# Stacked 128-row attention scores from copies in SBUF, and an earlier, partly moved conversion of q and k

## Chip, cores and metric

One core of one Trainium2 chip. The time is device microseconds of one execution; the kernel before takes 1062.03 us, the median of 3 runs (1060.99 to 1062.84).

## The reference

Three stages follow one another. Attention with 4 sink keys and a window of 128, over 4 batches x 8 heads x 768 positions x 64; an MLP with g = h - tanh(h); a mixture of 8 experts, of which each token takes one.

```python
scores = scale * np.matmul(q, k.transpose(0, 1, 3, 2))
keep = is_sink | in_window                 # 4 sink keys, and 0 <= i - j < 128
a = softmax(np.where(keep, scores, -1e9))
x = a @ v                                  # tokens 3072 x 512
h = x @ w_in;  y = (h - np.tanh(h)) @ w_out          # 512 -> 2048 -> 512
e = argmax(y @ w_gate + bias); out = gate * (relu(y @ w1[e]) @ w2[e])
```

## The kernel before

Every float32 product is made of float16 parts: x = hi + lo, and a product is lo*hi + hi*lo + hi*hi, accumulated in PSUM. Before the split, q and k of a group are scaled by a power of two found from their largest magnitude per partition (`qk_top_of`, L394: a reduction on VectorE; `qk_scales`, L405: eight small integer operations on VectorE, each followed by a wait for it; `qk_multiply`, L424: GpSimd multiplies in place; `conv`, L433: ScalarE writes hi, GpSimd writes lo = raw - hi).

Work is counted in pairs r = 0 to 95: one block of 128 queries of two heads. The two heads lie on partitions 0 to 63 and 64 to 127. Three pairs make a group g = r // 3 (384 queries), four groups a chunk of 384 tokens, and eight chunks are the whole; chunk m is also the token block of MLP window m. Each pair runs through `score_pair` (L566: six matmuls of 64 rows, three for each head, into two PSUM banks; VectorE masks and takes the maximum; ScalarE takes the exponential), `normalise`, `gather_sinks` (every third pair), `transpose_probs`, `transpose_sinks` (every third pair), `weigh_values` (64-column value products) and `split_x`. A block is 132 or 260 key columns wide: 132 where a sequence begins.

Pairs 0 to 13 are made in `alone` (L1270), two counts i = 2r and 2r + 1 for each pair, with the preparation of values and MLP weights (`prepare_alone`, L1171) between them. From pair 14 on they stand beside the MLP: `window` (L1315) has 32 slots k; even slots hold the first product of a hidden block (`mlp_in`, L756) and a pair, odd slots the second product (`mlp_out`, L816); four even slots of each window hold no pair. `between` puts the scores of a pair into the middle of the first product, after its xt_lo part. In window m the router of chunk m - 1 is worked (`gate_slot`, L963), the first part of its rank chain in slot 22.

`conversions` (L1154) says at which count i = 2r + (k mod 2) a group's reductions, scale and splits are issued. Groups 1 to 4 have counts of their own, group g from 5 on 6g - 9 (q top), 6g - 7 (k top, scale, multiply), 6g - 5 (q split), 6g - 3 (k split); its first pair is at count 6g. All engines run in order; every hand-over is a semaphore. SyncE (SP) issues the loads in the order written in `loads` (L1376): load_qk(g) waits until group g - 2 is converted, then in some places a value load with six small sink loads, or the store of a finished chunk.

Of the kernel before, what the change touches and what calls it, by code (L numbers as in the profile page):

```python
# [59 lines left out]
STRIP = 32  # L60
RING = 2
# [43 lines left out]
def attention_buffers(sb):  # L105
# [3 lines left out]
    k_hi, k_lo = ([sb(f"k_{x}{s}", [P, KR], F16) for s in range(2)] for x in ("hi", "lo"))  # L109
    v_raw = sb("v_raw", [P, NB2, DM], F32)  # L110
# [8 lines left out]
    words = 2 * QK + 2 * CT + 2 * KR + NB2 * DM + 2 * NB2 * HP * VW + 2 * DM + 2 * RING * KB + 6 * KB + 4 * SINK + P + 27 * P + 2 * RING * P  # L119
    return (qk_raw, q_hi, q_lo, k_hi, k_lo, v_raw, v_hi, v_lo, vs_raw, vs_all, probs, normed, sinks, pt, merged), words  # L120


def front(nc, dram, shared, attention):

    with ExitStack() as ctx:
# [6 lines left out]
        (qk_raw, q_hi, q_lo, k_hi, k_lo, v_raw, v_hi, v_lo, vs_raw, vs_all, probs, normed, sinks, pt,  # L132
# [35 lines left out]
        qk_top = sb("qk_top", [P, 2], F32)  # L168
# [22 lines left out]
        def h_of(m, f):  # L191
# [3 lines left out]
                 "qk_scaled qk_mult conv_hi conv_lo sink_zero sink_copied "  # L195
# [198 lines left out]
        def qk_top_of(E, eng, a, hp, i):  # L394

            g = HP * a + hp
            if E == "dve":
                if i == 0:
                    eng.wait_ge(q[f"qk_in{g % 2}"], 16 * (g // 2 + 1))
                elif g == 0:  # L400
                    eng.wait_ge(q["first_k_in"], 16)
                exponent_step(eng, eng.tensor_reduce(qk_top[:, i:i + 1], qk_raw[g % 2][:, qk_cuts(a)[i]], AX.X, ALU.max,  # L402
                                                     apply_absolute_value=True))

        def qk_scales(E, eng, a, hp):  # L405

            g = HP * a + hp
            if E == "dve":
                need(eng, q["qk_mult"], 2 * (g - 2))
                s = qk_scale[:, g % 2, :]  # L410
                for i in range(2):
                    one_exp = qk_exp[:, i:i + 1]
                    exponent_step(eng, eng.tensor_scalar(one_exp, qk_top[:, i:i + 1].bitcast(I32), 255 * EXP1, None,
                                                         ALU.bitwise_and))
                    exponent_step(eng, eng.tensor_scalar(one_exp, one_exp, float(LOWEST * EXP1), float(HIGHEST * EXP1),
                                                         ALU.max, ALU.min))
                exponent_step(eng, eng.tensor_scalar(qk_half[:], qk_exp[:, 1:2], qk_exp[:, 0:1], 0.5,
                                                     ALU.subtract, ALU.mult))
# [1804 lines left out]
```

## Time and profile before

| | |
|---|---|
| median of 3 runs | 1062.03 us |
| profiled execution, whole | 1065.34 us |
| its span, first to last instruction | 1063.4 us |
| TensorE (PE) busy | 979.7 us, 92% |
| VectorE (DVE) busy | 649.2 us, 61% |
| ScalarE (ACT) busy | 533.0 us, 50% |
| GpSimd (POOL) busy | 413.3 us, 39% |
| mean granted TensorE clock | 0.970 |

The profiled execution is 3.3 us above the median of the runs. PE's matmuls are pipelined: a row's duration overlaps the next row's, so the distance between starts tells what a matmul costs, not its duration. "PEld" are its weight loads.

### The profile page before, as it was taken

What the parts mean: (1) busy time and instruction counts of PE and PEld (TensorE: products, weight loads), DVE (VectorE), ACT (ScalarE), POOL (GpSimd) and SP (SyncE); (2) the same over time, 40 slices, a digit from 0 to 9 for tenths busy, and PEclk for the clock granted to TensorE, in tenths of its full rate; (3) what the DMA queues carried; (4) which work ended last, traced back from release to release, by engine and by line L of the source; (5) the groups of instructions that cost most, each with busy time, mean ns of one, the idle gap of its engine ahead of it and who ended that gap; (6) DMA issues with size and microseconds to landing.
All of it is one profiled execution on the core that took longest, in us unless ns stands there. A gap on an engine that the chain in (4) does not pass through costs nothing.

```text
span 1063.4 us, 23350 instructions
## 1 busy us (share of the span) xinstructions
PE 979.7 (92%) x7808; PEld 591.2 (56%) x7808; DVE 649.2 (61%) x1824; ACT 533.0 (50%) x1329; POOL 413.3 (39%) x605
## 2 busy tenths in 40 slices
PE   3647999999999999999999999999899999899996
PEld 2423444554554555555455455555576777677773
DVE  7565877767768767777866765547574324733331
ACT  4454776655646764655665555446512224522221
POOL 4555887524325533434642432200132322232322
PEclk9666999999999999999999999999999999999998
DMA  9502001102100212101110100051115112111111
GB/s 349 183 18 79 19 18 36 49 19 81 64 19 19 48 37 79 49 19 36 19 48 19 36 31 1 2 188 31 24 29 208 50 50 45 40 41 49 50 50 38
DMA packets 24371, 60.26 MB, mean 57 GB/s; under 512 B 9504, under 2 KB 9760, under 8 KB 22752
## 3 DMA queue, kind: packets, MB, share of 16 engines
q1 hardware_dynamic: 15392, 45.77, 13.2%
q0 software_dynamic: 5728, 13.43, 4.1%
q8 instruction: 44, 0.72, 0.3%
q10 hardware_dynamic: 3168, 0.02, 0.2%
q14 instruction: 39, 0.32, 0.1%
HBM read 45.35 MB, written 14.12 MB: 56 GB/s over the span
## 4 chain that ended last, share of the span: by engine, by line
PE 70%; DVE 14%; issue 5%; ACT 4%; POOL 3%; DMA 2%; DVEq 1%; ACTq 0%; POOLq 0%; SPq 0%
PE h_ps L772 18%; PE acc L828 18%; PE pt_ps L1897 5%; PE h_ps L1948 5%; PE acc L1948 5%; PE s_ps L1897 5%; PE s_ps L579 3%; PE x_out L727 3%; PE pt_ps L646 2%; PE s_ps L879 2%; DVE g_raw L793 1%; ACT probs L602 1%; ACT g_hi L803 1%; PE s_ps L772 1%; DVE qk_top L402 1%
## 5 line engine op out<-in xcount | busy, mean ns | idle before, releaser
L828 PE MATMUL acc<-w_out_all,g_hi 128*128 128x512 f16 x768 | 228.4, 379 | 0.0
L772 PE MATMUL h_ps<-xt_hi,w_in_all 128*128 128x384 f16 x960 | 197.5, 329 | 5.4 <-DVE g_raw L793 3.5
L828 PE MATMUL acc<-w_out_all,g_lo 128*128 128x512 f16 x384 | 146.0, 380 | 2.7 <-DVE g_lo L813 2.7
L772 PEld LDWEIGHTS h_ps<-xt_hi,w_in_all 128*128 128x128 f16 x960 | 91.0, 100 | 65.2 <-issue 8.6
L784 ACT ACTIVATE g_raw<-h_ps,batch_scale 128x384 f32<-128x384 f32 x120 | 69.6, 580 | 101.8 <-PE h_ps L772 101.8
L102 POOL TENSOR_TENSOR tick<-tick 1x1 f32<-1x1 f32 x83 | 15.5, 187 | 264.8 <-ACT y L1964 117.1
L828 PEld LDWEIGHTS acc<-w_out_all,g_hi 128*128 128x128 f16 x768 | 75.2, 98 | 77.7
L813 DVE SCALAR_TENSOR_TENSOR g_lo<-g_raw,batch_scale,g_hi 128x384 f16<-128x384 f32 x128 | 88.4, 690 | 41.9 <-ACT g_hi L803 40.5
L803 ACT ACTIVATE g_hi<-g_raw,batch_scale 128x384 f16<-128x384 f32 x128 | 79.0, 617 | 60.7 <-DVE g_raw L793 59.0
L661 POOL TENSOR_SCALAR_AFFINE_SELECT pt<-merged 128x512 f16<-128x512 f16 x96 | 65.3, 680 | 91.6 <-DVE merged L655 89.8
L772 PE MATMUL h_ps<-xt_lo,w_in_all 128*128 128x384 f16 x480 | 99.0, 329 | 0.0
L793 DVE SCALAR_TENSOR_TENSOR g_raw<-h_ps,batch_scale,g_raw 128x384 f32<-128x384 f32 x120 | 74.0, 617 | 38.4 <-ACT g_raw L784 35.7
L619 ACT ACTIVATE normed<-probs,row_sum 128x132 f32<-128x132 f32 x192 | 66.8, 395 | 31.0 <-DVE row_sum L613 22.2
L651 ACT ACTIVATE merged<-pt_ps 128x256 f16<-128x256 f32 x96 | 36.6, 382 | 75.7 <-PE pt_ps L646 75.2
L602 ACT ACTIVATE probs<-s_ps,neg_max 128x132 f32<-128x132 f32 x192 | 68.6, 365 | 6.4 <-DVE neg_max L596 6.2
L430 POOL TENSOR_SCALAR qk_raw<-qk_raw,qk_scale 128x384 f32<-128x384 f32 (+2 forms) x62 | 37.6, 618 | 75.1 <-DVE qk_scale L421 75.1
L772 PEld LDWEIGHTS h_ps<-xt_lo,w_in_all 128*128 128x128 f16 x480 | 47.4, 99 | 31.9 <-issue 1.4
L1861 ACT ACTIVATE xg<-xg,x_scale 128x512 f32<-128x512 f32 x23 | 16.6, 722 | 94.2 <-DVE x_undo L1858 94.2
L594 DVE COPY_PREDICATED s_ps<-later,s_ps 128x256 f32<-128x256 int32 x80 | 34.2, 428 | 47.6 <-PE s_ps L579 46.2
L451 POOL TENSOR_TENSOR q_lo<-qk_raw,q_hi 128x384 f16<-128x384 f32 x31 | 29.0, 934 | 83.5 <-ACT q_hi L447 83.4
L828 PEld LDWEIGHTS acc<-w_out_all,g_lo 128*128 128x128 f16 x384 | 37.5, 98 | 40.2 <-issue 5.2
L579 PE MATMUL s_ps<-k_hi,q_lo 64*128 64x260 f16 (+1 forms) x192 | 27.5, 282 | 31.0 <-ACT probs L602 21.7
(314 smaller groups left out, 2203.3 us busy)
## 6 DMA issues: line engine op xcount, KB each, us to landing
qk_raw<-in_qk SPq DMA_DIRECT2D x31, 454.0 KB, 3.3
raw<-in_w SPq DMA_DIRECT2D x16, 512.0 KB, 7.8
v_raw<-in_v SPq DMA_DIRECT2D x4, 1536.0 KB, 7.0
x_tokens<-x SPq DMA_DIRECT2D x24, 256.0 KB, 2.5
w_in_all<-in_w_in SPq DMA_DIRECT2D x4, 1024.0 KB, 8.8
w_out_all<-in_w_out SPq DMA_DIRECT2D x4, 1024.0 KB, 11.0
x_tokens<-g_raw SPq DMA_DIRECT2D x1, 1024.0 KB, 6.4
vs_raw<-in_v SPq DMA_DIRECT2D x24, 4.0 KB
```

The source lines that it names most:

```text
L579: mm = eng.matmul(s_banks[j][:, cols], l[s][rows, t * P:(t + 1) * P], k[s][rows, t * KB + cols.start:t * KB + KW], start=(i == 0), stop=(i ...
L602: eng.activation(probs[:, r % RING, j, :], s_banks[j][:, P:KW], ACT.Exp, bias=neg_max[:, r % RING, j:j + 1], scale=1.0, accum_out=row_sum[ ...
L619: eng.activation(normed[:, 2 * t + j, :], probs[:, r % RING, j, :], ACT.Copy, scale=row_sum[:, r % RING, j, 0:1])\
L661: eng.affine_select(out=at[:, :, 1, :], in_=both, pattern=[[0, 4], [1, P]], compare_op=ALU.is_ge, fill=0.0, base=0, channel_multiplier=-1) ...
L772: mm = eng.matmul(h_of(m, f), w16[0][:, f, x * DM + k * P:x * DM + (k + 1) * P], r[:, par, k, :], start=(i == 0), stop=(i == 3 * KD - 1))
L784: eng.activation(g_raw[:, f % 2, :], h_of(m, f), ACT.Tanh, scale=batch_scale[:, b, 0:1]).then_inc(q["tanh_done"], 1)
L793: eng.scalar_tensor_tensor(g, h_of(m, f), batch_scale[:, b, 0:1], g, ALU.mult, ALU.subtract).then_inc(q["g_done"], 1)
L803: eng.activation(g_hi[f % 2][:], g, ACT.Copy, scale=batch_scale[:, b, 1:2]).then_inc(q["g_hi_done"], 1)
L813: eng.scalar_tensor_tensor(g_lo[f % 2][:], g, batch_scale[:, b, 1:2], g_hi[f % 2][:], ALU.mult, ALU.subtract)\
L828: mm = eng.matmul(acc[t][:, :], l[f % 2][:, t * P:(t + 1) * P], w16[1][:, f, x * DM:(x + 1) * DM], start=(f == 0 and i == 0), stop=(f == N ...
L1897: mm = eng.matmul(hid_ps[c][:, (f - 4 * c) * P:(f - 4 * c + 1) * P], w[:, k, f * P:(f + 1) * P], x[p][:, k * P:(k + 1) * P], start=(i == 0 ...
L1948: mm = eng.matmul(y_ps[bank][:, :], l[:, f * P:(f + 1) * P], rhs, start=(f == 0 and i == 0), stop=(f == KF - 1 and i == 2))
```

## The change

Scores: from group 5 on (`STACKED = 5`) the operands are stacked to 128 rows, q as (q_hi, q_lo), the keys as (k_hi, k_hi) and (k_lo, k_lo). Two full-array matmuls for each head then give all four products, instead of three of 64 rows. The stacks are made by 12 DMA copies inside SBUF for each group, issued by SP before load_qk(g + 2). Conversions: the counts are earlier. Scale: qk_scales has five instead of eight operations, and runs on GpSimd for all groups but the first; qk_top has two buffers. In the alone part the value work moves: value scale and multiply earlier, value split and sink work later, weight Gram from count 5, sink transposes of ScalarE and VectorE one count later, first value products of a group one pair later in two places.

```diff
+STACKED = 5
+        q_stack = [sb(f"q_stack{s}", [P, 2, CT], F16) ...]; kh_stack, kl_stack: [P, 2, KR]
 def qk_top_of
-                exponent_step(eng, eng.tensor_reduce(qk_top[:, i:i + 1], ...))
+                need(eng, q["qk_scaled"], g - 1)
+                eng.tensor_reduce(qk_top[:, g % 2, i:i + 1], ...).then_inc(q["qk_topped"], 1)
 def qk_scales
-            if E == "dve":            # 8 operations, [P, 1] each
+            if E == ("pool" if g else "dve"):
+                step = chain(eng, q["qk_step"], QK_STEPS * g)
+                eng.wait_ge(q["qk_topped"], 2 * (g + 1))
+                need(eng, q["qk_mult"], 2 * (g - 2))
+                step(eng.tensor_scalar(qk_exp[:], qk_top[:, g % 2, :].bitcast(I32), 1.0 / EXP1, float(LOWEST), ALU.mult, ALU.max))
+                step(eng.tensor_scalar(qk_exp[:], qk_exp[:], float(HIGHEST), 0.0, ALU.min, ALU.add))
+                step(eng.tensor_scalar(qk_half[:], qk_exp[:, 1:2], qk_exp[:, 0:1], 0.5, ALU.subtract, ALU.mult))
+                step(eng.tensor_scalar(s[:, 0:1].bitcast(I32), qk_half[:], 127.0, float(EXP1), ALU.add, ALU.mult))
                 eng.tensor_scalar(s[:, 1:2]...).then_inc(q["qk_scaled"], 1)
+def stack_qk(E, eng, g):                # on SP
+                eng.wait_ge(q["conv_lo"], 2 * (g + 1))
+                eng.wait_ge(q["scores"], TPC * (g - 1))
+                for hh in range(2):
+                    for dst, part in (... six: q_hi, q_lo, k_hi twice, k_lo twice; 64 rows each ...):
+                        eng.dma_start(dst, part).then_inc(q[f"stacked{s}"], 16)
 def sink_halves
-                    eng.wait_ge(q["qk_mult"], 6)
+                    eng.wait_ge(q["conv_lo"], 8)
 def score_pair
+                if t == 0 and g >= STACKED:
+                    eng.wait_ge(q[f"stacked{s}"], stacked(g))
+                    for j in range(2):
+                        for i, k in enumerate((kl_stack, kh_stack)):
+                            mm = eng.matmul(s_banks[j][:, cols], q_stack[s][:, 1 - j, t * P:(t + 1) * P],
+                                            k[s][:, 1 - j, t * KB + cols.start:t * KB + KW], start=(i == 0), stop=(i == 1))
 def conversions
-                early = {1: (None, 0, 1, 2), 2: (4, 5, 7, 8), 3: (8, 9, 11, 12), 4: (14, 15, 17, 18)}
-                ... early.get(g, (6 * g - 9, 6 * g - 7, 6 * g - 5, 6 * g - 3))
+                early = {1: (None, 0, 1, 2), 2: (4, 5, 6, 7), 3: (8, 9, 10, 11), 4: (13, 14, 15, 16), 5: (19, 20, 21, 22)}
+                ... early.get(g, (6 * g - 11, 6 * g - 9, 6 * g - 7, 6 * g - 6))
 def prepare_alone
-            spread (PE) i == 5; v_scales, v_multiply 6; v_split 7; sink_multiply 8; sink_halves 9; weight_gram 4, 6, 7, 8
+            spread (PE) i == 4; v_scales 4 (DVE), v_multiply 5; v_split 8; sink_multiply 9; sink_halves 11; weight_gram 5, 6, 7, 8
 def alone
-            weighed = {5: (1,), 6: (2,), 7: (4, 5)}      # r: pairs weighed; (r - 2,) from 8 on
+            weighed = {5: (1,), 7: (2,), 8: (4, 5)}      # (r - 2,) from 9 on
+                    if i == 2 * r + (E in ("act", "dve")):   # was i == 2 * r for all
+                        stage(transpose_sinks, E, eng, r - 1)
 def loads
+                if g - 2 >= STACKED:
+                    stack_qk("sp", eng, g - 2)
                 load_qk("sp", eng, g)
+            stack_qk("sp", eng, HP * NC - 2)
+            stack_qk("sp", eng, HP * NC - 1)
```

## Rows read from the trace of the kernel before

**Rows 1.** Windows view: stretch, length, busy PE, PEld, DVE, ACT, POOL, clock, DMA.

```profile
8.40:88.40 80.00, 40.75 (x332) 27.30 (x332) 52.73 (x173) 41.45 (x131) 44.98 (x63) 0.72 0.47 176
88.40:187.00 98.60, 90.19 (x580) 44.77 (x580) 73.44 (x180) 65.90 (x171) 71.79 (x84) 0.95 0.08 25
187.00:765.00 578.00, 565.22 (x3767) 309.50 (x3764) 398.71 (x1114) 333.75 (x877) 209.94 (x290) 1.00 0.13 41
```

**Rows 2.** Timeline of PE, second window: start us, length, line, out<-in, shapes, count.

```profile
240.71 0.81 PE L772 MATMUL h_ps<-xt_lo,w_in_all 128*128 128x384 f16 x4
241.46 0.28 PE L579 MATMUL s_ps<-k_hi,q_lo 64*128 64x260 f16 x2
...
241.89 0.44 PE L646 MATMUL pt_ps<-ident,normed 128*128 128x128 f32 x2
...
245.61 0.81 PE L772 MATMUL h_ps<-xt_lo,w_in_all 128*128 128x384 f16 x4
246.26 0.38 PE L646 MATMUL pt_ps<-ident,normed 128*128 128x128 f32 x2
246.48 0.81 PE L772 MATMUL h_ps<-xt_hi,w_in_all 128*128 128x384 f16 x4
247.23 0.30 PE L727 MATMUL x_out<-pt,v_hi 128*64 128x256 f16 x2
...
250.26 0.52 PE L680 MATMUL pt_ps<-ident,sinks 128*128 128x128 f32 x3 [1.12 <-DVE merged L655]
...
250.83 0.59 PE L828 MATMUL acc<-w_out_all,g_hi 128*128 128x512 f16 x2
251.57 0.66 PE L772 MATMUL h_ps<-xt_hi,w_in_all 128*128 128x384 f16 x3
```

**Rows 3.** Timeline of PE: first score row of pairs 25, 27 and 30.

```profile
177.47 0.28 PE L579 MATMUL s_ps<-k_hi,q_lo 64*128 64x260 f16 x2
...
186.87 0.23 PE L579 MATMUL s_ps<-k_hi,q_lo 64*128 64x132 f16 x2
...
209.56 0.23 PE L579 MATMUL s_ps<-k_hi,q_lo 64*128 64x132 f16 x2
...
209.83 0.82 PE L772 MATMUL h_ps<-xt_hi,w_in_all 128*128 128x384 f16 x4
```

**Rows 4.** Timeline of PE's weight loads, alone stage at full clock.

```profile
54.65 0.92 PEld L293 LDWEIGHTS acc<-w_out_all 128*128 128x128 bf16 x16
```

**Rows 5.** SP's issue of six small loads; DMA view: size, us to landing.

```profile
243.83 2.36 SPq L472 DMA_DIRECT2D vs_raw<-in_v  x6
...
qk_raw<-in_qk SPq DMA_DIRECT2D x1, 192.0 KB, 2.4
slots<-table_fill SPq DMA_DIRECT2D x1, 192.0 KB, 6.9
```

**Rows 6.** Timeline of DVE: first and last of a group's eight scale operations.

```profile
246.84 0.15 DVE L413 TENSOR_SCALAR qk_exp<-qk_top 128x1 int32<-128x1 int32 x1
...
248.22 0.15 DVE L421 TENSOR_SCALAR qk_scale<-qk_scale 128x1 int32<-128x1 int32 x1
```

**Rows 7.** Waits of PE, 200 to 700 us, then 88 to 200: total, times, longest.

```profile
PE pt_ps L680 <- DVE merged L655: 5.0, 5, 1.1
...
PE pt_ps L680 <- DVE merged L655: 3.8, 4, 1.5
```

**Rows 8.** Groups of POOL by form: busy us, mean ns.

```profile
L102 POOL TENSOR_TENSOR tick<-tick 1x1 f32<-1x1 f32 x83 | 15.5, 187 | 264.8 <-ACT y L1964 117.1 <-DVE payload L951 66.7 <-DMA slot_g<-slots 40.4
...
L263 POOL TENSOR_SCALAR mod<-mod 128x24 f32<-128x24 f32 x1 | 0.4, 389 | 0.1
```

**Rows 9.** Timeline of ACT and POOL in the alone stage.

```profile
28.58 1.96 ACT L508 ACTIVATE v_hi<-v_raw 128x512 f16<-128x512 f32 x3 [1.94 <-POOL v_raw L493]
...
30.71 3.39 POOL L511 TENSOR_TENSOR v_lo<-v_raw,v_hi 128x512 f16<-128x512 f32 x3
...
36.29 0.63 ACT L525 ACTIVATE vs_all<-vs_raw 128x512 f16<-128x512 f32 x1 [3.04 <-POOL vs_raw L517]
```

More of the change, by code:

```diff
@@ L109, in attention_buffers @@
     k_hi, k_lo = ([sb(f"k_{x}{s}", [P, KR], F16) for s in range(2)] for x in ("hi", "lo"))
+    q_stack = [sb(f"q_stack{s}", [P, 2, CT], F16) for s in range(2)]
+    kh_stack, kl_stack = ([sb(f"k{x}_stack{s}", [P, 2, KR], F16) for s in range(2)] for x in ("h", "l"))
     v_raw = sb("v_raw", [P, NB2, DM], F32)
@@ L118, in attention_buffers @@
     merged = sb("merged", [P, RING, 2, 2, P], F16)
-    words = 2 * QK + 2 * CT + 2 * KR + NB2 * DM + 2 * NB2 * HP * VW + 2 * DM + 2 * RING * KB + 6 * KB + 4 * SINK + P + 27 * P + 2 * RING * P
-    return (qk_raw, q_hi, q_lo, k_hi, k_lo, v_raw, v_hi, v_lo, vs_raw, vs_all, probs, normed, sinks, pt, merged), words
+    words = 2 * QK + 4 * CT + 6 * KR + NB2 * DM + 2 * NB2 * HP * VW + 2 * DM + 2 * RING * KB + 6 * KB + 4 * SINK + P + 27 * P + 2 * RING * P
+    return (qk_raw, q_hi, q_lo, k_hi, k_lo, q_stack, kh_stack, kl_stack, v_raw, v_hi, v_lo, vs_raw, vs_all, probs, normed, sinks, pt, merged), words
 def front(nc, dram, shared, attention):
@@ L131, in front @@
         xt_hi, xt_lo = (sb(n, [P, 2, KD, CT], F16) for n in ("xt_hi", "xt_lo"))
-        (qk_raw, q_hi, q_lo, k_hi, k_lo, v_raw, v_hi, v_lo, vs_raw, vs_all, probs, normed, sinks, pt,
+        (qk_raw, q_hi, q_lo, k_hi, k_lo, q_stack, kh_stack, kl_stack, v_raw, v_hi, v_lo, vs_raw, vs_all, probs, normed, sinks, pt,
          merged) = attention
@@ L455, in conv, with stacked @@
                        .then_inc(q["conv_lo"], 1)
+        def stack_qk(E, eng, g):
+            s = g % 2
+            a = g // HP
+            k = key_cols(a)
+            if E == "sp":
+                eng.wait_ge(q["conv_lo"], 2 * (g + 1))
+                eng.wait_ge(q["scores"], TPC * (g - 1))
+                for hh in range(2):
+                    of_head = slice(D * hh, D * hh + D)
+                    upper, lower = slice(0, D), slice(D, P)
+                    for dst, part in ((q_stack[s][upper, hh, :], q_hi[s][of_head, :]),
+                                      (q_stack[s][lower, hh, :], q_lo[s][of_head, :]),
+                                      (kh_stack[s][upper, hh, k], k_hi[s][of_head, k]),
+                                      (kh_stack[s][lower, hh, k], k_hi[s][of_head, k]),
+                                      (kl_stack[s][upper, hh, k], k_lo[s][of_head, k]),
+                                      (kl_stack[s][lower, hh, k], k_lo[s][of_head, k])):
+                        eng.dma_start(dst, part).then_inc(q[f"stacked{s}"], 16)
+        def stacked(g):
+            return 16 * 12 * ((g - STACKED) // 2 + 1)
         def load_v(E, eng, b):
@@ L1280, in alone @@
                         score_pair(E, eng, r + 1)
[L1281 removed]
+                    for of in weighed.get(r, (r - 2,) if r > 8 else ()):
                         stage(weigh_values, E, eng, of)
@@ L1297, in alone @@
                         conversions(E, eng, i)
+                    if i == 2 * r + (E in ("act", "dve")):
+                        stage(transpose_sinks, E, eng, r - 1)
                     if i == 2 * r:
-                        stage(transpose_sinks, E, eng, r - 1)
-                        for of in weighed.get(r, (r - 2,) if r > 7 else ()):
+                        for of in weighed.get(r, (r - 2,) if r > 8 else ()):
                             stage(split_x, E, eng, of)
```

48 lines of the change are left out of this document (20 added, 28 removed).

## Prediction, made before the changed kernel was run

> **What bounds the kernel now.** I read the page first for the shares of the engines, then the windows view, which makes stages of the span [rows 1]: 8.4 to 88.4 us, 14 pairs scored "alone" (TensorE, PE, busy 40.8 of 80 us at a granted clock of 0.72); 88.4 to 187 us, the first MLP window (90.2 of 98.6); 187 to 765 us, the other windows (565.2 of 578 at full clock); then the experts, which the change leaves. In the windows a nanosecond off PE's own queue is a nanosecond off the span, and one off VectorE (DVE) counts only where PE waits for it. In the alone stage PE's own length hardly matters; the round trip ACT, PE, DVE does.
>
> Next PE's timeline in a window. A pair's scores stand between two parts of a hidden block. With them the transposes start 1.18 us after the xt_lo row (240.71 to 241.89); a slot later, without them, 0.65 us after (245.61 to 246.26) [rows 2]. So one pair's scores cost 0.53 us. The four matmuls of 384 columns in those 0.65 us give 0.423 ns a column, so 260 columns are 0.11 us; six such in 0.53 us cannot run one after another (0.66): the two 64-row halves run side by side, three passes, 0.33 us. The other 0.20 us is two pauses of 0.10: 240.71 + 0.65 = 241.36 against a first score at 241.46, and 241.46 + 0.33 = 241.79 against transposes at 241.89. The same pause stands ahead of the 64-column value products (246.48 + 0.65 = 247.13 against 247.23), and none ahead of full-array transposes that also wait for a semaphore (246.26) [rows 2]: it belongs to the change of array shape, not to the wait. The first block of a sequence has 132 columns and costs 0.10 + 0.27 (209.56 to 209.83) = 0.37 us [rows 3].
>
> **Edit 1, full-array scores for groups 5 and up.** 81 of the 96 pairs change: 69 with 260 columns, 12 with 132. Six half-array matmuls become four full ones, three passes become four: 4 x 0.11 = 0.44 us, and the pauses go, as the neighbours are full-array too. Gain 0.09 us, x69 = 6.2 us. For 132 columns the nearest row is the weight Gram, 16 matmuls of 128 columns whose weight loads take 0.92 us together, 0.058 each [rows 4]: 4 x 0.058 = 0.23, gain 0.14, x12 = 1.7 us. Together **7.9 us**. Bounds: 6.2 if the short blocks gain nothing because their weight loads show; about 0 if one pause of 0.10 us stays in every block (-8.1).
>
> The copies. Per group 12 copies of 64 partitions (49 to 67 KB each) on the SP queue. Six issues of L472 take 2.36 us, 0.39 each, so 4.7 us for 12; landing takes 2.4 us (192 KB of queries) up to 6.9 us (192 KB in small pieces) [rows 5]. So 7.1 to 11.6 us from k_lo to stacked; I take 7.1, since rows of 768 bytes and more are nearer the first. They start once k_lo of the group is made, now in the slot of the first pair of the group before, so by about that group's second pair, and are due at the next group's first pair. First pairs of groups 9 and 10 start 22.7 us apart (186.87, 209.56), a step from pair to pair is 4.7 (two steps from 177.47 to 186.87), so 18.0 us remain [rows 3]. The tightest place is group 9, its stretch having no pair-free slot: 177.47 to 186.87, 9.4 us, so 0 to 2.2 us late, once. I take 0. SP's queue: load_qk(g) now stands behind stack_qk(g-2), 4.7 us later, but both waited for the same k_lo, and its data is wanted a full group later; the MLP store that can hold SP ends with its window, when the next group's k_lo is only being made; load_v and its six sink loads stand behind a load that already waited. ACT's new q_hi may not overwrite before the scores of two groups back, already issued one slot earlier. All hidden by at least several us.
>
> The Trainium skill speaks against this edit: "TensorEngine Tiling (Array Packing)", Performance Considerations, asks for 2x row tiling at a contraction of 64, which the kernel gives up. By that rule a pair would go from three passes to four, 8.2 us dearer; that is rival C below. "DMA: Bandwidth & Descriptors", Rules for kernel authors, says of transfers under 64 KB that they are mostly overhead; no row here shows an SBUF to SBUF copy.
>
> **Edit 2, powers of two from DVE to POOL.** DVE loses eight instructions per group, 246.84 to 248.37, 1.53 us [rows 6]. Where does PE pay for them? Once in each of five windows they stand just ahead of the rank chain, the sink copy and merged, and PE's sink transposes wait 1.12 us for merged at 250.26; the hidden block behind them loses another 0.31 (250.83 + two matmuls of 512 columns, 0.43, to 251.57) as g_raw is late too [rows 2]. Five such waits in 200 to 700 us are 5.0 us [rows 7], with 5 x 0.31 it is 6.6. With the chain gone DVE is 1.53 us earlier there, a little more than PE loses (1.43), and k_top has moved two slots away. I take **6.5 us**; bounds 0 and 6.6. In the first window four more such waits are 3.8 us [rows 7]: I take **1.5 us**, bounds 4 and -3, because DVE and ACT also split weights there and POOL, busy 71.8 of 98.6 us [rows 1], takes the new chain.
>
> POOL's price: five small operations with a semaphore round each. Nearest rows: the one-element tick, 0.19 us, and a scalar operation of 24 columns, 0.39 us [rows 8]. With up to 0.08 us for the semaphore 5 x 0.27 = 1.4 us, bounds 1.0 and 2.4. Behind it queue the multiply, then v and w_out halves and the affine selects, whose readers are PE's value products. In the later windows POOL is busy 209.9 of 578 us [rows 1]: hidden. In the first window it is four more chains, 5.4 us on 71.8: inside the bound above.
>
> **Edit 3, the order in the alone stage.** Two waits hold ACT, and with it the exponential, the next scores and DVE: v_hi for the values' multiply (1.94 us at 28.58, then 1.96 us of work ahead of the next exponential) and vs_all for the sinks' multiply (3.04 us) [rows 9]. The change puts value work later and multiplies earlier, so both should shrink: up to 5.0 us. But q_hi of groups 3, 4 and 5 now comes one or two slots earlier, right behind k_top, so ACT will wait for POOL's chain and multiply instead (k_top end + 1.4 + 0.6 us), and for group 3 that chain stands behind the three v_lo, 3.39 us on POOL [rows 9]. Stepping through the pairs with these durations I find exponentials up to 3.7 us earlier in the middle and nearly level by pair 12, whose ACT waits for v_hi of the last block, itself behind k_lo on POOL. I take **0**, bounds -5 and +3.4.
>
> **Sum**, against the profiled execution (1065.34 us, span 1063.4): -7.9 - 6.5 - 1.5 + 0 = -15.9, so 1049.4. The median of the runs shown is 1062.03, 3.3 lower, so 1046.1: I say **1046**.
>
> **Rivals.**
> A. DVE's relief is given back: the rank chain alone still delays the sinks, or POOL's chain delays its selects in the first window. For it: the rank chain and the sink copy stay where they are. Against it: DVE gains 1.53 us there and PE lost 1.43. Only edit 1 counts: 1054.
> B. The alone stage keeps its gains, 4 to 5 us: 1041. For it the two waits; against it ACT's new waits.
> C. The pauses belong to the score block as such, or the stacked matmuls pause too: block 0.64 instead of 0.53, four passes instead of three, +8.2 in place of -7.9, and with the DVE gains 1062, no change. Against it the pauses around the value products and their absence at 246.26.
> D. The copies come late, slower than before: each of 27 groups waits. The slack in a normal group is 18.0 us; the gain is gone from about 18.6 us for twelve copies (15.9 / 27 = 0.6 us late each). At 19.8 us each group is 1.8 late: 1062 - 16 + 49 = 1095. Against it: far over my figure and above the upper bound of 11.6.
>
> **Chances.** Forecast 0.58 (own range 1042 to 1051), A 0.16, B 0.10, C 0.07, D 0.09. A measurement of this kernel can tell about 0.2% (2 us) from no change. Faster: forecast, A and B, 0.84; same: most of C, 0.06; slower: D and the rest of C, 0.10. The range of 8 in 10 takes in A and B and their bounds: 1038 to 1058; C and D (0.16) lie outside.
>
> **What would show it.** In PE's timeline of a window: xt_lo to transposes 1.09 us instead of 1.18, four score matmuls 0.11 apart, no 0.10 before them (edit 1). PE's wait for merged before the sink transposes near zero in the windows (edit 2); if it stays at 1 us per window, A. MLP's first matmul still near 88 us (edit 3); near 84, B. A wait of PE's first score matmul of a group for a DMA: D. Wrong altogether if PE is no longer what the windows wait for.

## The result, and the profile after

The changed kernel takes 1051.26 us (median of 5 runs, 1049.43 to 1052.9) against 1062.03 for the kernel before on the same chip (1058.94 to 1064.4): a ratio of 0.9897, interval 0.9879 to 0.9915, or 10.8 us less. Forecast were 15.9 us less. The profiled execution took 1051.26 us, its span is 1049.7.

I cut both traces at the same points of the work (PE's first MLP product; PE's first weight load of each later window) and take distances of starts. Values in us:

| stage | before | after | forecast change | measured |
|---|---|---|---|---|
| to the first MLP product | 88.4 | 88.8 | 0 | +0.4 |
| from there to the end of the first window | 96.8 | 96.1 | -2.7 | -0.8 |
| windows 2 to 7 | 509.7 | 498.7 | -13.2 | -11.0 |
| last window, no pairs | 70.2 | 70.2 | 0 | 0 |
| experts, code unchanged | 298.3 | 295.9 | 0 | -2.4 |

The 13.2 is edit 1's part for the pairs there (about 6.7) and edit 2's 6.5; the 2.7 is the rest of edit 1 (1.2) and 1.5. In other profiles of this study the unchanged experts took 294.2 to 298.3 us; the six windows of one program repeat to 0.1 us (509.68 and 509.69 in two profiles of the kernel before). So the windows are where an effect can be read, and the last row of the table is noise. The first two rows scatter too, by up to 4.4 us between executions of nearly the same code; e3 and e4 below show it.

The stages in the windows view (stretch, length, busy PE, PEld, DVE, ACT, POOL, clock, DMA share, GB/s), first of the kernel before, cut where its second window and its experts begin, which [rows 1] does only roughly:

```profile
88.40:185.30 96.90, 88.49 (x566) 43.89 (x567) 71.94 (x177) 64.20 (x167) 70.35 (x81) 0.95 0.08 25
185.30:765.10 579.80, 567.02 (x3778) 310.38 (x3776) 400.21 (x1117) 335.45 (x881) 211.48 (x294) 1.00 0.13 41
```

Then of after, at the same points of the work:

```profile
8.80:88.80 80.00, 37.51 (x328) 24.90 (x326) 45.43 (x133) 42.09 (x131) 52.42 (x89) 0.76 0.48 179
88.80:184.90 96.10, 86.33 (x542) 46.77 (x543) 67.65 (x145) 63.89 (x166) 75.41 (x104) 0.95 0.19 50
184.90:753.70 568.80, 556.95 (x3639) 324.62 (x3638) 378.75 (x940) 334.43 (x881) 239.53 (x399) 1.00 0.25 69
```

DVE lost 4.3 us of work in the first window (71.94 to 67.65) and POOL gained 5.1 (70.35 to 75.41); in the later windows DVE lost 21.5 and POOL gained 28.1. The DMA share there about doubled, 0.13 to 0.25: the copies.

A pair's scores in a hidden block, PE's timeline of after (start, length, line, out<-in, shapes, count):

```profile
240.41 0.81 PE L805 MATMUL h_ps<-xt_lo,w_in_all 128*128 128x384 f16 x4
241.06 0.27 PE L612 MATMUL s_ps<-kl_stack,q_stack 128*128 128x260 f16 x1
241.17 0.27 PE L612 MATMUL s_ps<-kh_stack,q_stack 128*128 128x260 f16 x1
241.28 0.28 PE L612 MATMUL s_ps<-kl_stack,q_stack 128*128 128x260 f16 x1
241.39 0.27 PE L612 MATMUL s_ps<-kh_stack,q_stack 128*128 128x260 f16 x1
241.50 0.38 PE L679 MATMUL pt_ps<-ident,normed 128*128 128x128 f32 x2
...
245.88 0.81 PE L805 MATMUL h_ps<-xt_hi,w_in_all 128*128 128x384 f16 x4
246.62 0.30 PE L760 MATMUL x_out<-pt,v_hi 128*64 128x256 f16 x2
```

From xt_lo to the transposes it is 1.09 us (240.41 to 241.50) where it was 1.18 [rows 2]. The first score comes 0.65 us after xt_lo, with no pause, and the four are 0.11 apart. The pause ahead of the 64-column value products is still there (245.88 + 0.65 = 246.53, they start at 246.62).

The gain goes on behind the transposes. In the kernel before the next product starts 0.28 us after them (241.89 [rows 2] to 242.17):

```profile
242.17 0.81 PE L772 MATMUL h_ps<-xt_hi,w_in_all 128*128 128x384 f16 x4
```

In after the product behind the transposes of 241.50 starts 0.22 us later:

```profile
241.72 0.81 PE L805 MATMUL h_ps<-xt_hi,w_in_all 128*128 128x384 f16 x4
```

0.22 us is also what the same transposes take in the kernel before where no scores stand ahead of them (246.26 to 246.48 [rows 2]). So a block with scores and transposes went from 1.46 to 1.31 us (240.71 to 242.17, 240.41 to 241.72): 0.145 us between the medians of the 46 such blocks of windows 2 to 7. It is 0.09 in the 12 that have scores of 260 columns and no transposes, and 0.144 in ten of the eleven 132-column ones (the eleventh waits for its copies). Together that is about 9.3 us off PE's own queue (46 x 0.145 + 12 x 0.09 + 11 x 0.144, the eleventh by estimate).

Where PE still waits, 200 to 700 us of after (us in total, times, longest):

```profile
PE pt_ps L713 <- DVE merged L688: 2.6, 5, 0.7
PE pt_ps L679 <- ACT normed L652: 1.5, 2, 0.8
PE s_ps L912 <- DVE row_top L332: 1.4, 2, 0.7
PE h_ps L805 <- DVE g_raw L826: 0.8, 2, 0.4
```

The wait for merged was 5.0 us in five [rows 7] and is 2.6 in five, but these are not the same five. Before, the sink transposes of groups 11, 15, 19, 23 and 27 waited, those behind the rank chain (at 250.26, 337.65, 421.72, 509.10 and 593.18 us). Of these only 15 and 23 still wait, 0.36 and 0.37 us instead of 0.81 each; 11, 19 and 27 (1.1 each) do not. Three waits are new, at groups 9, 17 and 25, early in windows 2, 4 and 6 (0.58, 0.67 and 0.67 us), where the kernel before had none:

```profile
206.79 0.52 PE L713 MATMUL pt_ps<-ident,sinks 128*128 128x128 f32 x3 [0.58 <-DVE merged L688]
```

So of the 5.0 us 4.3 went where the prediction looked for it, and 1.9 came elsewhere. The waits for normed (0.5 before) and g_raw (0.4 before) have grown. The row_top wait is as it was, 1.4.

In the first window (88.5 to 190 us) the merged waits have gone too: three of the four of [rows 7], 3.2 of its 3.8 us (the fourth, at 190.64 us, is in the second window). These stand there:

```profile
PE x_out L760 <- POOL pt L697: 4.2, 3, 2.7
PE h_ps L805 <- DVE g_raw L826: 3.7, 4, 1.5
PE h_ps L805 <- DVE xt_lo L785: 1.2, 1, 1.2
PE s_ps L612 <- DMA kl_stack<-k_lo: 1.1, 1, 1.1
```

### The profile page after: what moved, and what is told of

The parts are those of the page before. It is cut to its first block, busy times and chain, and to the rows that moved or that the text cites. A ratio compares the mean times of both kernels' runs of the same rounds, so it can differ in the third digit from the quotient of the medians.

```text
span 1049.7 us, 23285 instructions
## 1 busy us (share of the span) xinstructions
PE 963.0 (92%) x7646; PEld 605.3 (58%) x7646; DVE 617.0 (59%) x1573; ACT 532.2 (51%) x1329; POOL 454.1 (43%) x760
## 4 chain that ended last, share of the span: by engine, by line
PE 69%; DVE 9%; POOL 8%; issue 6%; ACT 4%; DVEq 1%; DMA 1%; SPq 1%; ACTq 0%; POOLq 0%
PE acc L861 18%; PE h_ps L805 17%; PE h_ps L1986 5%; PE s_ps L1935 5%; PE pt_ps L1935 5%; PE acc L1986 5%; PE x_out L760 3%; PE s_ps L612 3%; PE s_ps L912 2%; PE pt_ps L679 1%; POOL pt L694 1%; POOL v_lo L536 1%; POOL v_raw L518 1%; POOL qk_raw L432 1%; PE x_out L1912 1%
## 5 line engine op out<-in xcount | busy, mean ns | idle before, releaser
L694 POOL TENSOR_SCALAR_AFFINE_SELECT pt<-merged 128x512 f16<-128x512 f16 x96 | 67.6, 704 | 107.3 <-DVE merged L688 107.0
L453 POOL TENSOR_TENSOR k_lo<-qk_raw,k_hi 128x524 f16<-128x524 f32 (+1 forms) x31 | 33.2, 1072 | 101.2 <-ACT k_hi L449 101.1
L688 DVE TENSOR_TENSOR merged<-pt_ps,merged 128x256 f16<-128x256 f32 x96 | 39.9, 416 | 34.9 <-ACT merged L684 34.7
L697 POOL TENSOR_SCALAR_AFFINE_SELECT pt<-merged 128x512 f16<-128x512 f16 x80 | 54.5, 681 | 0.0
## 6 DMA issues: line engine op xcount, KB each, us to landing
w_out_all<-in_w_out SPq DMA_DIRECT2D x4, 1024.0 KB, 13.2
```

The lines of the kernel that those rows point to most:

```text
L694: eng.affine_select(out=at[:, :, 1, :], in_=both, pattern=[[0, 4], [1, P]], compare_op=ALU.is_ge, fill=0.0, base=0, channel_multiplier=-1) ...
L697: eng.affine_select(out=at[:, :, 0, :], in_=both, pattern=[[0, 4], [-1, P]], compare_op=ALU.is_gt, fill=0.0, base=0, channel_multiplier=1) ...
```

## Experiments

All times are medians of 4 to 12 runs beside runs of the kernel before on the same chip, but for e5, a single run. Times of kernels on different chips are compared by their ratios to the kernel before, the changed kernel's being 0.9897 (0.9879 to 0.9915). "First part" is the time up to the end of the first MLP window (before 185.3, after 184.9), "windows" the sum of windows 2 to 7 (before 509.7, after 498.7); both come from one profile of each kernel.

The first part has a scatter of its own, and PE's granted clock is in it. In every profile the clock is 0.50 at the first MLP product and rises to 1.00 during the next ones, either 3.3 to 4.0 us after that product (e1, e3, e6, e7, e9) or 8.2 to 9.3 us after it (the nine others, before and after among them). The second product comes 8.4 to 8.7 us behind the first one in the former and 9.9 to 10.4 in the latter, 1.5 us apart.

**The score form alone.** e1 has everything but the stacks:

```diff
-STACKED = 5
+STACKED = 32
 def loads
-                if g - 2 >= STACKED:
-                    stack_qk("sp", eng, g - 2)
```

e2 makes the copies and waits for them, but computes the scores from the 64-row halves:

```diff
 def score_pair
-                if g < STACKED:
+                if True:
                     for i, (l, k) in enumerate(((q_lo, k_hi), (q_hi, k_lo), (q_hi, k_hi))):
```

> The changed kernel with all scores in the old form (six 64-row matmuls) and no copies; conversions, GpSimd scale and alone order stay new. My theory, that the stacked form is worth 0.09 us on each of 69 pairs and 0.14 on 12 (7.9 us, less 1.3 for the one late group seen in the trace, 6.6): 3 to 5 us faster than the kernel before, that is 6 to 8 slower than the changed kernel, a score block of 0.53 us, and no 1.27 us wait before pair 27. Rival: the gain came from the vector engine alone and the form is worth nothing: as fast as the changed kernel, 10 to 11 us faster than before.

> The changed kernel with the 12 copies and the wait for them kept, but the scores computed in the old 64-row form from the unstacked operands. It separates the form from the copies. My theory: the copies cost only the one late group (1.3 us), so it is 0.5 to 2 us slower than the kernel without copies (e1), 2 to 4 us faster than before. Rival: copies beside the MLP slow other things (loads, the engines' reads): 3 us or more slower than e1, equal to before.

Measured: e1 1060.43 us, ratio to before 0.9995 (0.9984 to 1.0007), windows 505.59; e2 1060.84, ratio 1.0000 (0.9991 to 1.0009), windows 505.57. So form and copies together are worth 505.59 - 498.72 = 6.9 us in the windows, where 6.7 of the forecast's 7.9 lie. Without the one late group it is 8.0 (e8 below, 497.61). By the ratios the whole kernel is 10.4 us slower without them (1.0 per cent), more than the 6 to 8 expected. e1 and e2 agree to 0.02 us in the windows: the copies' traffic and their issue on SP cost PE nothing there. The late group of after does not show in e2, whose first window ends 2.4 us later, so that the copies land in time.

The surprise is that e1 and e2 are level with the kernel before, where 3 to 5 and 2 to 4 us less were expected, though their windows are 4.1 us shorter (509.68 to 505.59). The profiles show a part of what was lost: their first parts are 186.6 and 187.2 us against 185.3 and 185.6 (e5), 1 to 2 us more. The other 2 to 3 us are in no stage of the profiles whose code was changed, and stay open. What stands in the first part:

```profile
167.31 0.30 PE L760 MATMUL x_out<-pt,v_hi 128*64 128x256 f16 x2 [2.67 <-POOL pt L697]
...
167.99 1.05 PE L861 MATMUL acc<-w_out_all,g_hi 128*128 128x512 f16 x2
168.83 0.63 PE L861 MATMUL acc<-w_out_all,g_lo 128*128 128x512 f16 x1
```

These rows are e1's PE timeline: a wait of 2.67 us for POOL, then matmuls of 512 columns 0.42 us apart (168.83 - 167.99 = 0.84 for two; at full clock 0.43 for two). The windows view from there on (stretch, length, busy times, clock, DMA share, GB/s):

```profile
168.00:171.40 3.40, 3.40 (x11) 1.70 (x10) 0.36 (x1) 1.53 (x3) 3.39 (x5) 0.50 0.02 5
171.40:180.00 8.60, 8.10 (x61) 4.19 (x60) 5.30 (x11) 4.22 (x13) 4.69 (x5) 1.00 0.00 0
```

The granted clock was 0.50, the 1.2 GHz level, for 3.4 us after the pause. The profile of after has the same 2.67 us wait and no such stretch behind it. What a stretch costs can be read from four kernels whose code is the same from there on but for e8's earlier copies: from the end of this wait to the end of the first window it is 17.5 us in after and e6, without a stretch, and 19.0 in e8 and e9, with one: 1.5 us.

**The powers of two.** e3 has the new five-operation chain, but on VectorE for all groups; e4 on VectorE up to group 9 and on GpSimd after:

```diff
 def qk_scales
-            if E == ("pool" if g else "dve"):
+            if E == "dve":                              # e3
+            if E == ("pool" if g > 9 else "dve"):       # e4
```

> The changed kernel with the five scale operations of every group on the vector engine again. Theory: the 2.3 us chain on GpSimd made its selects late in the first window (value products wait 4.7 us there, 2.8 in one place), and the later windows gain from its absence on the vector engine. So the first window gets 2 to 4 us shorter, the later windows 1 to 3 us longer (5 operations of 0.19 us, 0.95 us a group, away from the rank chain), in all within 2 us of the changed kernel. Rival: the move itself is what gained 4 us in the windows: windows 1 to 6 4 us or more longer.

> Scale on the vector engine for groups 0 to 9 (alone stage and first window), on GpSimd from group 10 on. Theory: it takes the first window's gain of e3 and keeps the later windows of the changed kernel: 2 to 5 us faster than the changed kernel, 13 to 15 faster than before; the alone stage within 2 us of 88.8. Rival: the first window's value products wait for something else than the chain (w_out halves on GpSimd): no difference from the changed kernel.

Measured: e3 1053.62 us, ratio 0.9939 (0.9927 to 0.9952), windows 504.01; e4 1047.76, ratio 0.9877 (0.9861 to 0.9893), windows 498.27. With the new counts the move is worth 504.01 - 498.72 = 5.3 us in the windows, so the rival of e3's expectation came true; by the ratios e3 is 4.5 us slower than the changed kernel. What came back with the chain on VectorE, PE's waits of e3, 200 to 700 us:

```profile
PE h_ps L805 <- DVE g_raw L826: 4.3, 5, 0.9
PE s_ps L612 <- DVE logit L921: 2.8, 5, 0.9
```

No wait for merged is left in e3; five for g_raw and five for the router's logit stand instead. So the earlier counts (with five operations instead of eight) alone took VectorE's chain away from merged, and put it ahead of other readers; only together with the move to GpSimd do they gain. The counts without the move and without the stacks were not run. In the first window of e4 the wait for GpSimd is 1.1 us instead of 4.2, but VectorE's are longer:

```profile
PE h_ps L805 <- DVE g_raw L826: 5.5, 4, 1.5
PE s_ps L325 <- ACT probs L635: 2.0, 1, 2.0
PE pt_ps L679 <- ACT normed L652: 1.5, 2, 0.8
PE x_out L760 <- POOL pt L697: 1.1, 1, 1.1
```

That profile also holds a 3.4 us stretch at half clock at 140 us, behind a wait of 2.0 us, and is the slowest of e4's four runs (1052.76). Its first part was 185.5 us, no shorter than that of after. e3's was 181.1, 3.8 us under after's and in the range that e3's expectation gave, though up to group 9 the code is the same: its first MLP product came at 86.0 us and not 87.5, its clock rose 4.0 us after that and not 8.2, and the same 2.0 us wait has no half-clock stretch behind it. That is 4.4 us between two executions of the same code but for group 10's chain in the last 10 us: a first part of one profile tells nothing finer. By the ratios e4 is 2.1 us faster than the changed kernel, with overlapping intervals, so whether the chain should leave GpSimd in the first window is not shown by e4.

**The kernel before again, unchanged** (e5), for the scatter of a stage.

> The kernel before, unchanged, profiled once more, because its first profile has a dip of the granted clock at 913 us in the expert stage and ran 3.3 us above the median. Expected: windows 1 to 6 again 509.7 us (they repeat to 0.1 in the traces so far), the rest after 765 us about 296.5 instead of 298.3, and the start of the MLP's second product, 98.7 before, 1 to 3 us earlier; if it is 98.7 again, the alone stage of the changed kernel costs nothing.

Measured: 1061.54 us. First part 185.6 (185.3 in the first profile), windows 509.69 (509.68), experts 294.2 (298.3). The first profile has two half-clock stretches of 3.4 us in the experts, at 913 and 1050 us, and this one has neither. At 1.5 us each (the price found above) they are 3 of the 4.1 us between the two, and most of why the first profile stood 3.3 us above its median.

**The alone stage in its old order, with all else changed** (e6):

```diff
 def conversions
-                early = {1: (None, 0, 1, 2), 2: (4, 5, 6, 7), 3: (8, 9, 10, 11), 4: (13, 14, 15, 16), 5: (19, 20, 21, 22)}
+                early = {1: (None, 0, 1, 2), 2: (4, 5, 7, 8), 3: (8, 9, 11, 12), 4: (14, 15, 17, 18), 5: (19, 20, 21, 22)}
 def prepare_alone                # and alone(): counts of spread, v, sinks, Gram as before the change
```

> The changed kernel with the order of the alone stage as before (conversion counts of groups 1 to 4, value scale, multiply and split, sinks, weight Gram, sink transposes, pairs weighed), the scale on GpSimd and the stacked scores kept. My theory: the new order is worth nothing net, within 2 us of the changed kernel either way. Rival 1: the new order saves the two waits, 5 us: 3 to 5 us slower than the changed kernel. Rival 2: the scale on GpSimd needs the old order's slack: faster by 2 or more.

Measured: 1051.56 us, ratio 0.9911 (0.9891 to 0.993), first part 185.7, windows 498.15. In the whole time the new order is worth nothing that can be measured, as forecast. At the first MLP product it is: 91.3 us with the old order against 88.8. In the first part 0.8 us of this is left, but there e6's clock rose 3.5 us after that product and after's 8.7, which gave e6 about 1.5 us back.

**The old lead of the conversions, with the stacks** (e7):

```diff
 def conversions
-                ... early.get(g, (6 * g - 11, 6 * g - 9, 6 * g - 7, 6 * g - 6))      # 5: (19, 20, 21, 22)
+                ... early.get(g, (6 * g - 9, 6 * g - 7, 6 * g - 5, 6 * g - 3))       # 5 by the same rule
```

> The changed kernel with the counts of groups 5 and up as before (6g-9, 6g-7, 6g-5, 6g-3) and the stacks kept: k_lo comes three slots before it is due, not six. From k_lo to the last copy landed is 9.0 us in the trace (235.68 to 244.66); three slots are 7 to 9 us and 12 with a pair-free slot between. Theory: PE waits 1 to 4 us for the copies before the first pair of most groups, 30 to 60 us in all, which would be slower than the kernel before; it also puts k_top ahead of the rank chain again. Rival: slots stretch elsewhere and the copies cost little: within 5 us of the changed kernel.

Measured: 1062.5 us, ratio 1.0019 (1.0002 to 1.0037), windows 511.30. The copies come late, 88.5 to 190 us and then 190 to 700:

```profile
PE s_ps L612 <- DMA kl_stack<-k_lo: 8.9, 4, 5.1
```

```profile
PE s_ps L612 <- DMA kl_stack<-k_lo: 9.9, 11, 1.9
```

18.8 us of waiting at the first score of a group. The windows lose 12.6 us against after, more than the stacks gave. I had expected 30 to 60 us of waiting; the slots between k_lo and the first pair are nearly as long as the copies. The run moves k_top back as well, and does not separate the two. Against that its alone stage ended 5 us earlier (84.8 us), which pointed to group 5, whose counts it also moves (tried alone in e9).

**Copies as soon as each half is made** (e8), with the powers of two on VectorE up to group 5:

```diff
 def stack_qk
-                eng.wait_ge(q["conv_lo"], 2 * (g + 1))
-                for hh in range(2): ... twelve copies
+                for stage_ in range(3):      # q_hi, q_lo; k_hi; k_lo: four copies each
+                    eng.wait_ge(*((q["conv_lo"], 2 * g + 1), (q["conv_hi"], 2 * g + 2), (q["conv_lo"], 2 * g + 2))[stage_])
+                    for hh in range(2): ... the copies of that part
 def qk_scales
-            if E == ("pool" if g else "dve"):
+            if E == ("pool" if g > 5 else "dve"):
```

> Two changes to the changed kernel: the scale of groups 1 to 5, the alone stage's, on the vector engine and on GpSimd from 6 on; and the copies of q issued as soon as q_lo is made, those of k_hi as soon as k_hi is. Theory: the alone stage gets 1 to 3 us shorter as in e3 and e4, and the wait of 1.27 us before pair 27 goes as its copies land 2.5 us earlier: 2 to 4 us faster than the changed kernel, 13 to 15 faster than before. Rival: the alone stages of e3 and e4 were chance: only the 1.3 us.

Measured: 1049.1 us, ratio 0.9881 (0.9859 to 0.9903), windows 497.61. PE no longer waits for a copy; the window in which group 9 begins went from 83.98 to 82.72 us. What VectorE's chain for groups 1 to 5 brought is not shown: the first MLP product came at 87.6 us instead of 88.8, in the first part nothing is left of that (185.4; a half-clock stretch of 1.5 us is in it), and the ratio is within the changed kernel's interval. The wait for GpSimd in the first window (4.4 us, 4.2 in after) belongs to group 9, which has its chain on GpSimd in both.

**Group 5 later** (e9), and then all three together (e10):

```diff
-                ... 5: (19, 20, 21, 22)}
+                ... 5: (21, 23, 25, 27)}
 def qk_scales                                           # e10 only, with e8's stack_qk
-            if E == ("pool" if g else "dve"):
+            if E == ("pool" if g not in (0, 9) else "dve"):
```

> The changed kernel, with group 5 converted at slots 21, 23, 25, 27 instead of 19, 20, 21, 22 and nothing else moved. My theory (from the run with the old lead, whose alone stage ended 5 us earlier): in the changed kernel ACT waits 2.75 us for POOL before q_hi of group 5 and has that conversion ahead of the last values of the alone stage, so moving it brings the first MLP load to 84 to 86 us instead of 88.8 and the time 2 to 4 us down; the windows from the second on stay at 498.7 us in sum. Rival: the 5 us were scatter between executions of an unchanged stage (runs with the same alone stage stood 85.0 to 89.5): then the first MLP load stays at 87 to 89 and the ratio to the changed kernel's is within 0.2%. Second rival: the later k_lo of group 5 makes the first stacked copies late for pair 15, and the first MLP window gives back 1 to 3 us.

> The version that the runs so far point to: copies issued as each half is made, group 5 later as in the run beside it, and the powers of two of group 9 alone on VectorE (GpSimd has the others). Theory: the 1.27 us wait of group 9's first score matmul goes, and with the chain of 2.3 us off GpSimd in the crowded part of the first window the values' wait for pt there shrinks from 2.7 to about 1.2 us; together 2.5 to 3 us under the run with group 5 alone moved, so 1044 to 1046 us where the kernel before has 1061. Rival: the chain on VectorE gives as much back in that window as in the two runs with it there so far, and only the 1.3 us of the copies are left.

Measured: e9 1048.83 us, ratio 0.9877 (0.985 to 0.9905); e10 1043.17, ratio 0.9822 (0.98 to 0.9845). e9's first MLP product starts at 84.4 us, as expected, instead of 88.8. This is not scatter: in the four profiles with group 5 later (e7, e9, e10, e12) it starts at 84.4 to 85.2 us, in the eight of kernels with the changed kernel's counts for group 5 at 86.0 to 91.3. In the whole time e9 alone stays within noise of the changed kernel (0.9877 against 0.9897). ACT's timeline of after shows what went:

```profile
69.20 0.52 ACT L449 ACTIVATE q_hi<-qk_raw 128x384 f16<-128x384 f32 x1 [2.75 <-POOL qk_raw L432]
...
78.26 0.63 ACT L533 ACTIVATE v_hi<-v_raw 128x512 f16<-128x512 f32 x1 [4.17 <-POOL v_raw L518]
```

The second rival came true as well: pair 15's scores wait 1.11 us for the copies of group 5 in e9 (at 97.32 us), and it gives back a part. In e10 neither wait for a copy is left, and GpSimd's in the first window is smaller (88.5 to 190 us of e10; after's are above):

```profile
PE x_out L761 <- POOL pt L698: 2.6, 3, 1.2
```

e9 has a half-clock stretch right behind its 2.7 us wait for GpSimd (its granted clock is 0.78 from 160 to 165 us and 0.88 from 165 to 170); e10, whose wait there is 1.06 us, has 1.00 in both. The first part is 181.4 us in e9 and 179.6 in e10, the windows 498.60 and 497.57. So e10 gained more than the 2.5 to 3 us expected, 5.7 us by the medians, of which its profile shows 2.8 in these stages and 2.0 in the unchanged experts, which is scatter. In the first part e9 has the half-clock stretch and e10 the later rise of the clock behind the first MLP product, about 1.5 us each way.

**q_hi and q_lo one slot earlier** (e11: from group 6 on; e12: from group 10 on, with all of e10):

```diff
-                ... early.get(g, (6 * g - 11, 6 * g - 9, 6 * g - 7, 6 * g - 6))
+                ... early.get(g, (6 * g - 11, 6 * g - 9, 6 * g - 8, 6 * g - 6))                        # e11
+                ... early.get(g, (6 * g - 11, 6 * g - 9, 6 * g - (8 if g > 9 else 7), 6 * g - 6))      # e12
```

> The changed kernel with q_hi and q_lo of each group from 6 on one slot earlier (6g-8 instead of 6g-7). It asks where the 4.1 us against the 6.5 forecast for VectorE's relief went: theory: into q_hi, which now stands on ScalarE in the slot whose merged the sink transposes wait for (0.53 to 0.84 us in five windows, and 0.57 us twice in the hidden block behind). With q_hi a slot earlier these waits go and windows 2 to 7 take 495.5 to 496.5 us instead of 498.7, if nothing replaces them. Rival: any slot has a reader whose turn comes late on ScalarE (normed, 0.93 us in two windows, stands in such a slot already), so the stalls only move: sum within 1 us of 498.7, or above it.

> The version with early copies, group 5 later and group 9's powers of two on VectorE, and q_hi and q_lo one slot earlier from group 10 on (not before: in the first window group 9's earlier q_hi waited 2.56 us for GpSimd on ScalarE, and PE's transposes 3.0 us for normed behind it). Theory: the two effects are in different windows and add: windows 2 to 7 go from 497.6 to 494.6 us, the first stays at 84.4, the time from 1043.2 to about 1040.2. Rival: the gain of 3.0 us in the windows leans on GpSimd having made qk_raw in time, or is taken back by other waits once the copies start earlier; then 1043 or more.

Measured: e11 1054.15 us, ratio 0.9925 (0.9904 to 0.9945), windows 495.71, first part 188.4; e12 1042.42, ratio 0.9822 (0.9807 to 0.9838), windows 495.50, first part 179.2. PE's waits of e11, 200 to 700 us, have no merged among them:

```profile
PE s_ps L912 <- DVE row_top L332: 1.4, 2, 0.7
PE pt_ps L679 <- ACT normed L652: 1.3, 4, 0.5
PE h_ps L805 <- DVE g_raw L826: 0.7, 2, 0.4
```

That names the cause of the five that after has. Ahead of the one at group 15 (POOL's timeline, then ACT's):

```profile
326.39 0.23 POOL L417 TENSOR_SCALAR qk_exp<-qk_top 128x2 int32<-128x2 int32 x1
...
328.00 1.16 POOL L432 TENSOR_SCALAR qk_raw<-qk_raw,qk_scale 128x384 f32<-128x384 f32 x2
329.12 0.94 POOL L694 TENSOR_SCALAR_AFFINE_SELECT pt<-merged 128x512 f16<-128x512 f16 x1
...
330.64 0.69 POOL L518 TENSOR_SCALAR v_raw<-v_raw,v_scale 128x512 f32<-128x512 f32 x1
```

```profile
331.36 0.63 ACT L533 ACTIVATE v_hi<-v_raw 128x512 f16<-128x512 f32 x1 [2.00 <-POOL v_raw L518]
331.89 0.51 ACT L449 ACTIVATE q_hi<-qk_raw 128x384 f16<-128x384 f32 x1
332.31 0.36 ACT L684 ACTIVATE merged<-pt_ps 128x256 f16<-128x256 f32 x1
```

GpSimd's chain and multiply hold its queue from 326.39 to 329.12; the values' multiply waits behind them and two selects, ScalarE waits 2.00 us for it, does v_hi and q_hi, and only then its half of merged; VectorE's half waits for that, and PE's sink transposes (333.27) for VectorE's. All five are alike: each time ScalarE has waited 1.8 to 2.2 us for GpSimd's v_raw, 1.9 to 2.4 us earlier. Moving q_hi (0.42 us from start to start) out of this place ended all five waits, 0.36 to 0.67 us each. The gain in the windows is 3.0 us in e11, but only 2.07 from e10 to e12: in e11 about 1 us of it is group 9's copies, which the longer first window hid. In the first window the same move cost more than it gave. e11 there, at 168.57 us:

```profile
168.57 0.69 PE L679 MATMUL pt_ps<-ident,normed 128*128 128x128 f32 x2 [3.05 <-ACT normed L652]
```

It stands behind ScalarE's own 2.56 us wait for qk_raw ahead of q_hi. e12 keeps group 9 where it was and is the shortest kernel of the study, though 1040.2 us and windows of 494.6 were expected: 1.8% under the kernel before; its median is 0.75 us under e10's, on another chip, and the two ratios are equal, so that its last step shows in the windows of the profiles only.

## Why the prediction was right or wrong

**Edit 1: the mechanism right, the size met with luck.** 7.9 us forecast, 6.7 of it in the windows; measured 6.9 there. To the transposes 1.09 us, four matmuls 0.11 apart, no pauses: each as forecast. Rival C (pauses stay) is out. But the sum stopped at the transposes, and a long block gains another 0.055 us behind them (0.28 to 0.22): 9.3 us in the windows and not 6.7. The prediction's own rows held the sign, 246.26 to 246.48 without scores ahead. Of the 9.3, 1.3 went to the late copies of group 9, taken as 0, and most of the rest to longer waits for merged and normed (e8, whose copies are in time, keeps 8.0). That two errors nearly cancel is luck. By the whole times of e1 nearly all of the change's gain is this edit: 10.4 of 10.8 us (to about 2 us, by the intervals), where 7.9 of 15.9 were forecast. The Trainium skill's rule of 2x row tiling at a contraction of 64 ("TensorEngine Tiling (Array Packing)", Performance Considerations) did not hold as advice here: stacked was faster by those 6.9 us, since each change of array shape between full-array neighbours had cost 0.10 us and the full-array transposes behind the 64-row scores another 0.055.

**The copies: priced too low, still mostly hidden.** Issue was put at 0.39 us each; it is 0.64. SP's timeline for one group:

```profile
235.68 0.46 SPq L476 DMA_DIRECT2D q_stack<-q_hi  x1
...
236.82 1.24 SPq L476 DMA_DIRECT2D kh_stack<-k_hi  x2
...
241.95 1.24 SPq L476 DMA_DIRECT2D kl_stack<-k_lo  x2
```

235.68 to 243.2 is 7.5 us instead of 4.7, and the last copy landed 9.0 us after k_lo instead of 7.1, inside the bound of 11.6. This group is among the quickest: over the 27 groups the issue takes 7.5 to 10.0 us, 8.7 for group 9. At the tightest place, named in advance, this made PE wait:

```profile
187.67 0.23 PE L612 MATMUL s_ps<-kl_stack,q_stack 128*128 128x132 f16 x1 [1.11 <-DMA kl_stack<-k_lo]
```

185.74 + 0.65 = 186.39 against 187.67: 1.28 us, once, in the range of 0 to 2.2 of which I had taken 0. e8 removes it. Everywhere else the longer lead hides the copies. e7 shows that the stacks do not pay without it: that is rival D's mechanism, at 18.8 us of waiting.

**Edit 2: the relief right, its price missed.** In the windows I took 6.5 us; e1 against before, which has edit 2 and the earlier counts without the stacks, shows 4.1. The waits behind the rank chain went as forecast, 5.0 us to 0.7 in after at the same five places. The step that failed is the term for GpSimd in the later windows, "hidden", that is 0. The queue behind the chain was followed to the value products only; the reader that mattered was the values' multiply, then v_hi and merged on ScalarE, and the moved q_hi stood in the same place. The price is 2.6 us of waits for merged (1.9 at three new places, 0.7 at two old ones) and the longer ones for normed and g_raw. e11 and e12 show it: without q_hi there no wait for merged is left, and the windows are 2.1 to 3.0 us shorter. The chain itself takes 1.6 us in the windows (326.39 to 328.00) where I took 1.4; its bound of 2.4 was reached in the first window:

```profile
162.54 0.23 POOL L417 TENSOR_SCALAR qk_exp<-qk_top 128x2 int32<-128x2 int32 x1
162.86 0.65 POOL L418 TENSOR_SCALAR qk_exp<-qk_exp 128x2 int32<-128x2 int32 x1
163.61 0.66 POOL L419 TENSOR_SCALAR qk_half<-qk_exp 128x1 int32<-128x1 int32 x1
...
164.95 1.16 POOL L432 TENSOR_SCALAR qk_raw<-qk_raw,qk_scale 128x384 f32<-128x384 f32 x2
```

162.54 to 164.95 is 2.4 us, then the multiply and the selects, and PE's value products wait 2.67 us at 167.35. So in the first window the merged waits of 3.2 us went and 4.2 us for GpSimd came: the 1.5 us of relief and edit 1's 1.2 us together left 0.8, a size that one profile can't tell from scatter. The prediction read [rows 7] as four waits of 3.8 us in this window; one of them, 0.55 us at 190.64, is in the next. The exchange is the second half of rival A, that GpSimd's chain delays its selects in the first window. Its first half, that the rank chain alone delays the sinks as before, is out: e3, e11 and e12 have no wait for merged in the later windows.

**Edit 3: level as forecast, by a cancellation not foreseen in full.** As the prediction said, waits were exchanged: up to the first MLP product ScalarE waits 11.3 us for q_hi's input from GpSimd in after, which the kernel before did not wait for, while the 3.0 us for vs_all went and v_hi's 7.4 us became 6.2. But "level" hides two larger terms: the new order puts the first MLP product 2.5 us earlier (e6, one profile), and group 5's earlier counts, which my stepping through the pairs did not price, put it 4 us later (e7, e9, e10, e12). Rival B's 84 us is what a better order gives.

**The sum.** Of 15.9 us, 11.4 show outside the experts in the profiles and 10.8 in the medians. Missing are about 2.2 us in the windows (edit 2's 6.5 measured 4.1; edit 1's two errors nearly cancel) and 2.3 us in the first part, within its scatter. The time, 1051.26, lies within the range of 8 in 10 and 0.3 us above the forecast's own (1042 to 1051); rival A said 1054.

## What to carry to other kernels

Where 64-row matmuls stand between full-array ones, measure the distance of starts around them, up to the block behind the next one: four stacked passes beat three half-array ones because of the pauses, and the copies are free only if their whole chain (issue, landing) fits between the conversion and the first reader. When work moves to a less busy engine, follow everything queued behind it there, through each reader, to the bounding engine: a share of 36% (209.9 of 578 us) said "hidden", and the queue at five places did not. When a wait shrinks, look where it stands: five before and five after were mostly different ones. Judge steps of this size by stages that repeat, not by whole-kernel times that scatter by 2 to 4 us.

## What the runs showed of the hardware

- The granted clock fell to 0.50 for 3.4 us within 1.2 us of the end of a PE wait of 2.7 to 2.8 us in the first window in e1, e2, e7, e8 and e9, and not in after and e6, with the same wait; behind a wait of 2.0 us it did so in e4 and not in e3. Such a stretch costs 1.5 us. It makes a wait dearer than its length, but not each time.
- Behind the first MLP product the granted clock rose from 0.50 to 1.00 after 3.3 to 4.0 us in five profiles and after 8.2 to 9.3 us in nine, with the same code on both sides (e3, e4); the second product then comes 1.5 us later.
- Two full-array transposes behind 64-row matmuls take 0.28 us to the next product, behind full-array ones 0.22.
- Two operations of one or two elements a partition on GpSimd took 0.65 us in the first window (162.86 and 163.61) and 0.23 and 0.32 in a later one (326.71 and 327.04); which neighbour stretched them was not tried.
- A copy inside SBUF of 64 partitions (48 to 66 KB) took SP 0.60 to 0.64 us to issue in most groups and 2.0 to 2.1 us (medians) to land; twelve of them took 7.5 to 10.0 us to issue.
